# Layer 1 in pairs of tiles with seven block products each, layer 2's weights in layer 1's places, and a cosine without the absolute value

## What is computed

```python
X = rfft(x, axis=1)                  # x: 2 x 3008 x 256, an FFT layer with a complex 256x256 mix
Yr, Yi = Xr @ w_r - Xi @ w_i + b_r, Xr @ w_i + Xi @ w_r + b_i
Y = soft_threshold(Yr, 0.01) + 1j * soft_threshold(Yi, 0.01)
x = irfft(Y).reshape(6016, 256)
h = x @ w_in;  x = (h * cos(h)) @ w_out                        # layer 1: 256 -> 2048 -> 256
h = x @ w_in2; y = (h * clip(h + 3, 0, 6) / 6) @ w_out2        # layer 2: 256 -> 2048 -> 256
```

## Time and profile before

| | us |
|---|---|
| median of 3 runs (1182.27 to 1183.05) | 1182.86 |
| the profiled execution | 1183.26 |
| its span from first to last instruction | 1181.2 |
| PE busy | 1166.5 |
| ACT, DVE, POOL busy | 773.1, 760.9, 748.8 |
| mean granted TensorE clock | 0.998 of full speed |

### The profile page before, as it was taken

How to read it: one execution, slowest core, us unless ns; L and a number is a source line. 1 busy time by engine, 2 the same in 40 slices (tenths; PEclk the granted TensorE clock), 3 DMA queues, 4 the chain that set the end, 5 groups by cost and what they waited for, 6 DMA issues and landing times.

```text
span 1181.2 us, 15354 instructions
## 1 busy us (share of the span) xinstructions
PE 1166.5 (99%) x5432; PEld 985.4 (83%) x5432; DVE 760.9 (64%) x827; ACT 773.1 (65%) x1100; POOL 748.8 (63%) x505
## 2 busy tenths in 40 slices
PE   8999979999999999999999999999999999999998
PEld 8888869888888888888888888888888888888898
DVE  2777826677777777777777766565465465555544
ACT  2677656656666666666666667767667676676665
POOL 2577656556767777565677559957657557557544
PEclk9999999999999999999999999999999999999999
DMA  9375537100100100101010021020010100100000
GB/s 251 124 199 156 139 90 277 32 19 18 36 19 19 36 18 19 36 32 54 23 36 1 18 67 41 1 73 1 12 61 1 37 36 1 67 1 1 37 1 32
DMA packets 32793, 62.58 MB, mean 53 GB/s; under 512 B 3585, under 2 KB 11393, under 8 KB 32568
## 3 DMA queue, kind: packets, MB, share of 16 engines
q1 hardware_dynamic: 32718, 61.61, 16.9%
HBM read 37.22 MB, written 24.48 MB: 52 GB/s over the span
## 4 chain that ended last, share of the span: by engine, by line
PE 97%; DMA 1%; DVE 0%; ACT 0%; POOL 0%; issue 0%; SPq 0%
PE banks L627 22%; PE banks L685 22%; PE banks L644 21%; PE banks L666 19%; PE banks L519 2%; PE banks L539 2%; PE banks L535 2%; PE banks L534 2%; PE banks L592 2%; PE banks L555 1%; PE banks L554 1%; DMA v<-y_spill 1%; PE banks L504 1%; PE banks L570 0%; PE banks L567 0%; PE banks L568 0%
## 5 line engine op out<-in xcount | busy, mean ns | idle before, releaser
L1339 POOL TENSOR_TENSOR gal<-ga,gah 128x1024 fp32r<-128x1024 f32 (+1 forms) x95 | 250.0, 2632 | 174.8 <-ACT gah L897 173.3
L1420 POOL TENSOR_TENSOR gbl<-gb,gbh 128x512 fp32r<-128x512 f32 (+1 forms) x192 | 249.9, 1313 | 168.8 <-ACT gbh L1028 168.4
L889 ACT ACTIVATE cosine<-phase,half_pi 128x1024 f32<-128x1024 f32 (+1 forms) x96 | 108.8, 1133 | 132.8 <-DVE phase L1152 132.7
L1197 DVE SCALAR_TENSOR_TENSOR gb<-ramp,banks 128x512 f32<-128x512 f32 (+1 forms) x144 | 97.0, 674 | 143.1 <-ACT ramp L1021 143.1
L1170 DVE TENSOR_TENSOR ga<-banks,cosine 128x1024 f32<-128x1024 f32 (+1 forms) x96 | 115.4, 1202 | 113.4 <-ACT cosine L889 113.4
L1028 ACT ACTIVATE gbh<-gb 128x512 fp32r<-128x512 f32 (+1 forms) x192 | 118.5, 618 | 58.5 <-DVE gb L1197 57.9
L1152 DVE TENSOR_SCALAR phase<-phase 128x1024 int32<-128x1024 int32 (+1 forms) x96 | 152.7, 1590 | 3.3
L685 PE MATMUL banks<-gbh,w_lo 128*128 128x512 f32 (+1 forms) x384 | 147.9, 385 | 0.0
L685 PE MATMUL banks<-gbl,w2h 128*128 128x512 f32 (+1 forms) x384 | 147.9, 385 | 0.0
L685 PE MATMUL banks<-gbh,w2h 128*128 128x512 f32 (+1 forms) x384 | 147.9, 385 | 0.0
L666 PE MATMUL banks<-th,w2h 128*128 128x512 f32 (+1 forms) x336 | 129.4, 385 | 0.0
(11 more groups left out here) (104 smaller groups left out, 2189.6 us busy)
## 6 DMA issues: line engine op xcount, KB each, us to landing
w<-in_w_ff SPq DMA_DIRECT2D x32, 256.0 KB, 4.9
xb<-in_x SPq DMA_DIRECT2D x32, 192.0 KB, 5.7
y_spill<-y SPq DMA_DIRECT2D x24, 256.0 KB, 2.0
x<-x_spill SPq DMA_DIRECT2D x11, 512.0 KB, 4.0
x_spill<-x SPq DMA_DIRECT2D x11, 512.0 KB, 3.0
x_spill<-xs SPq DMA_DIRECT2D x11, 470.0 KB, 3.6
t<-x_spill SPq DMA_DIRECT2D x10, 512.0 KB, 4.6
out_y<-yt SPq DMA_DIRECT2D x10, 512.0 KB, 3.1
```

Of the source, the lines that this page charges most:

```text
L889: act.activation(cosine[:, :, 0:w], phase[G % 2][:, :, 0:w], ACT.Sin, bias=half_pi[:, :], scale=-1.0).then_inc(a_cos, 1)
L1339: pool.tensor_tensor(gal[G % 2][:, :, 0:w], ga[G % 2][:, :, 0:w], gah[G % 2][:, :, 0:w].bitcast(fp32), ALU.subtract).then_inc(a_gl, 1)
L1420: pool.tensor_tensor(gbl[n % RING][:, 0:w], gb[n % G_BUFS][:, 0:w], gbh[n % RING][:, 0:w].bitcast(fp32), ALU.subtract).then_inc(b_gl, 1)
```

## The change

- Layer 1 keeps the old form for its first two tiles (16 steps). The other ten are taken as five duos, 40 steps of the layer-2 kind, ahead of layer 2's six duos. In these 40 steps a block goes through `take_turns2` (ACT), `take_angle2` (DVE), `take_cos2` (ACT), `take_g2` (DVE), `round_gb` and `gb_low`, each 512 wide, in place. `copy_u2` is on DVE. The last two tiles' results of each duo go through `copy_y` (ACT) and `take_y` (DVE).
- The sums of layer 1's weight blocks are made in the 16 old steps: raw blocks loaded, `sum_s` on POOL, `round_s` on ACT, `s_low` on DVE, one pair a step. The first duo's data are prepared there too.
- Layer 2's eight weight pairs are loaded into layer 1's places as each comes free, in the last duo of layer 1 and the first of layer 2 (`load_w2`, `sum_w2`, `round_w2`, `w2_low`).
- The turns are made with a bias of -0.25, and the absolute value (L1152) goes, in all steps of layer 1.
- `sum_t` moves from two in step p = 1 and one each in p = 2, 3 to one each in p = 1 to 4, on DVE ahead of the last `take_angle2`. PSUM banks and the rings of buffers change (g: 8 and 6).

```diff
-STEPS1 = TILES * PAIRS
-DUOS = -(-TOKENS // (2 * TOK))
+CLASSIC = 2
+STEPS1 = CLASSIC * PAIRS
+DUOS1 = (TILES - CLASSIC) // 2
+DUOS2 = -(-TOKENS // (2 * TOK))
+DUOS = DUOS1 + DUOS2
+CHANGE, STEPS2 = DUOS1 * PAIRS, DUOS * PAIRS
...
             def load_w2(p):
-                sp.dma_start(w2f[p][:, A11:A11 + 4 * P], w_ff[NWCH + 2 * p, :, :]).then_inc(w2_in[p], 16)
-                sp.dma_start(w2f[p][:, UP2:W2COLS], w_ff[NWCH + 2 * p + 1, :, :]).then_inc(w2_in[p], 16)
+                freed(sp, 4 * (CHANGE - PAIRS + p) + 3)
+                for part in range(2):
+                    at = p * PCOLS + part * WCH
+                    sp.dma_start(w1f[:, at:at + WCH], w_ff[NWCH + 2 * p + part, :, :]).then_inc(w2_in[p], 16)
...
-                act.activation(phase[G % 2][:, :, 0:w].bitcast(i32), bank[:, at:at + 2, 0:w], ACT.Copy,
-                               scale=1.0 / (2.0 * math.pi)).then_inc(a_turns, 1)
+                act.activation(phase[G % 2][:, :, 0:w].bitcast(i32), bank[:, at:at + 2, 0:w], ACT.Identity,
+                               bias=quarter[:, :], scale=1.0 / (2.0 * math.pi)).then_inc(a_turns, 1)
...
+            for s in range(CHANGE):                      # ACT
+                q, p = divmod(s, PAIRS)
+                keep_u1(s)
...
+                    take_cos2(s - 1, 3)
+                keep_u5(s)
+                take_turns2(s, 0)
...
+                    round_gb(s - 1, 3)
+                if s == 1:
+                    copy_x2(1)
+                prepare2(s)
+                take_cos2(s, 0)
+                take_turns2(s, 1)
+                round_gb(s, 0)
+                take_turns2(s, 2)
+                take_cos2(s, 1)
+                take_cos2(s, 2)
+                round_gb(s, 1)
+                take_turns2(s, 3)
+                if p == 0 and q >= 1:
+                    copy_y(q - 1, 0)
+                    copy_y(q - 1, 1)
+                round_gb(s, 2)
...
-                dve.wait_ge(a_angle, G + 1)
-                bits = angle[:, :, 0:w].bitcast(i32)
-                dve.tensor_scalar(bits, bits, 0x7FFFFFFF, None, ALU.bitwise_and).then_inc(a_abs, 1)
...
+            def take_angle2(s, i):
+                n = 4 * s + i
+                dve.wait_ge(b_turns, n + 1)
+                g = gb[n % RING_G]
+                dve.scalar_tensor_tensor(out=g[:, :], in0=g[:, :].bitcast(i32), scalar=-2.0 * math.pi,
+                                         in1=h_block(s, i), op0=ALU.mult, op1=ALU.add).then_inc(b_angle, 1)
+
+            def take_g2(s, i):
+                n = 4 * s + i
+                dve.wait_ge(b_cos, n + 1)
+                g = gb[n % RING_G]
+                dve.tensor_tensor(g[:, :], h_block(s, i), g[:, :], ALU.mult).then_inc(b_g, 1)
...
+            for s in range(CHANGE):                      # DVE
+                q, p = divmod(s, PAIRS)
+                take_c11(s)
...
+                    take_g2(s - 1, 3)
+                copy_u2(s)
+                take_angle2(s, 0)
+                take_c12(s)
+                take_g2(s, 0)
+                take_c22(s)
+                take_angle2(s, 1)
+                take_angle2(s, 2)
+                take_g2(s, 1)
+                take_g2(s, 2)
+                prepare2(s)
+                take_angle2(s, 3)
+                if p == 0 and q >= 1:
+                    take_y(q - 1, 2)
+                    take_y(q - 1, 3)
```

More of the change, by code:

```diff
@@ L127, in mixer_program @@
         three = small.place("three", [P, 1], fp32)
+        quarter = small.place("quarter", [P, 1], fp32)
         sine_table = small.place("sine_table", [P, 1], fp32)
@@ L173, in mixer_program @@
         assert r.at <= nc.sbuf_usable_end
-        w2h, w2f, w2l = [None] * PAIRS, [None] * PAIRS, [None] * PAIRS
+        r = Region(v_at)
+        sh, sf, sl = [None] * PAIRS, [None] * PAIRS, [None] * PAIRS
+        for p in range(PAIRS):
+            sh[p] = r.place(f"sh{p}", [P, 4 * P], f32r)
+        for p in range(PAIRS):
+            sf[p], sl[p] = twice(r, f"s{p}", [P, 4 * P])
+        x2 = r.place("x2", PAIR, fp32)
+        ga1_at = r.at
+        ga.append(r.place("ga1", PAIR, fp32))
+        gbh_at = r.at
@@ L176, in mixer_program @@
+        xs.append(Region(gbh_at).place(f"xs{SBUF_X}", [P, DC, SPILL], fp32))
+        raw = [r.place(f"raw{i}", [P, 4 * P], fp32) for i in range(RAWS)]
+        assert r.at <= w1_at
+        r = Region(gbh_at)
+        gbh = [r.place(f"gbh{i}", ONE, f32r) for i in range(RING_H)]
+        assert r.at <= w1_at
         th, tf, tl = [None] * 2, [None] * 2, [None] * 2
[L177 to L180, removed]
+        r = Region(work_at)
@@ L192, in mixer_program @@
[L192 to L213, removed]
+        tf[0], tl[0] = twice(r, "t0", [P, 7, TOK])
@@ L214, in mixer_program @@
+        u1, u2, u5 = r.place("u1", ONE, fp32), r.place("u2", ONE, fp32), r.place("u5", ONE, fp32)
+        c22 = r.place("c22", ONE, fp32)
+        gb, gbl = [None] * RING_G, [None] * RING_G
+        gb[0], gbl[0] = twice(r, "gb0", ONE)
+        assert r.at <= nc.sbuf_usable_end
+        r = Region(u_at)
+        for i in range(1, 5):
+            gb[i], gbl[i] = twice(r, f"gb{i}", ONE)
+        yt = r.place("yt", [P, 2, DC, TOK], fp32)
+        assert r.at == phase_at
         th[1] = r.place("th1", [P, 7, TOK], f32r)
@@ L215, in mixer_program @@
         tf[1], tl[1] = twice(r, "t1", [P, 7, TOK])
+        gb[7], gbl[7] = twice(r, "gb7", ONE)
         assert r.at <= v_at
+        r = Region(ga1_at)
+        for i in range(5, 7):
+            gb[i], gbl[i] = twice(r, f"gb{i}", ONE)
         bank = ctx.enter_context(nc.psum_tensor("banks", [P, 8, 512], fp32))
@@ L1258, in _ @@
                 take_angle(G + 1)
-            for s in range(STEPS2):
+                prepare1(G)
+            for s in range(CHANGE):
                 q, p = divmod(s, PAIRS)
@@ L1268, in _ @@
                 take_gb(s, 2)
-                if p == 0 and q >= 1:
+                if p == 0:
                     take_y(q - 1, 0)
```

550 lines of the change are left out of this document (307 added, 243 removed).

## The result

The kernel after takes 1185.02 us (median of 14 runs, 1182.44 to 1185.69), the kernel before, beside it, 1182.49 (14 runs, 1181.64 to 1183.44). The ratio is 1.0019, 95% interval 1.0011 to 1.0027: the change costs about 0.2%, where 1176 was forecast, 0.6% less. The profiled execution took 1185.33 us with a span of 1183.5, against 1183.26 and 1181.2 of before: +2.3 us in the span.

A forecast was written before the change was run, and what follows sets the result against it. PE, busy in 99% of the span, was taken to bound the kernel. Sum: 1183.26 - 27.2 (matmuls) + 18.1 (duo stalls) + 0.5 (old steps) + 1.6 (layer change) = 1176.3, less 0.4 for the median: 1176 us; range 1160 to 1191.

The forecast's parts named there:

- the 120 matmuls and their pace: Layer 1's ten tiles on PE: 1800 matmuls instead of 1920, at 0.2267 us each, 27.2 us less.
- the stalls of the duos: Layer 1's five duos: loops above PE's 10.2 us make PE stall, 3.3 us a usual duo, 18.1 in all.
- The 1.3 extra of the last duo: Last layer-1 duo, steps 5 to 7: five `round_w2` and a `w2_low` add 1.3 us to its 3.3.
- the sums slip in ahead of POOL: Rival: in p = 1 to 3 DVE's `sum_t` goes before POOL's remainder; 1164 us; chance 0.28, shared with stalls smaller still.
- every loop is longer: Rival: hand-overs and POOL's lock cost 0.5 us more in each of forty steps; 1190 us, slower; chance 0.16.
- The duo's preparation lies in steps of 5.4 us with room.: First duo's data prepared in the old steps ahead of step 0: room enough, no cost put in the sum.
- the change of layers: Step 40: four `round_w2` and a cosine ahead of `keep_u2` make it late for p7, 1.6 us.
- Steps 43 to 46 ... nothing, at most 0.2 each.: Steps 43 to 46: four extra roundings where before had three with 0.7 us to spare; at most 0.2 each.
- The clock: Rival: granted clock falls after PE stalls; called small, stalls being at most 1.7 us in a 10.2 step; no chance given.
- Old steps: The 16 old steps: `sum_s` puts four instructions, 2.1 us, on POOL; stall 0 to 1.4 us, 0.5 taken.
- The cosine: Layer 1's turns: dropping DVE's absolute value is worth nothing by itself; the bias's 83 ns are hidden in old steps.
- something at the seams is late: Rival: weights or first duo's data late by one or two steps, 1186 us at most; chance 0.12 with the space between.

The follow-up runs named there:

- Experiment 5: Kernel after with `sum_t` of duos 1 to 5 replaced by writes of zeros that read nothing: 1172.02 us, ratio to before 0.9911.
- 6: Kernel after with `sum_t` moved behind `take_angle2` of block 3, all work kept: 1172.60 us, ratio to before 0.9914.
- experiment 1: Kernel after with T4's remainder made on DVE after step 13 instead of on POOL: 1179.63 us, ratio to before 0.998.
- experiment 2: Kernel after with `w2_low` of the second weight pair ahead of step 40's own ramps on DVE: 1180.05 us, ratio to before 0.9981.
- Experiment 4: Kernel after with 13 useless matmuls filling PE's wait ahead of step 0: 1183.01 us, ratio to before 1.0008.
- experiment 7: Kernel before with only the turns' bias of -0.25 and no absolute value: 1182.41 us, ratio to before 0.9999.
- experiment 8: Kernel after with T4's remainder on DVE, the second pair's `w2_low` earlier and `sum_t` later: 1163.49 us, ratio to before 0.9837.
- experiment 9: Kernel of experiment 8 with `w2_low(0, 2)` moved between step 39's angles of blocks 1 and 2: 1162.88 us, ratio to before 0.9835.

## Why the prediction was wrong

**Right: the 120 matmuls and their pace.** 5312 are there, 12 of them in 2.72 us. 27.2 us went off PE.

**Right, a little large: the stalls of the duos.** The mechanism is as worked out: POOL goes in between the g of c22 and `sum_t`, PE waits on `keep_u5`, and p = 6 catches up (9.73). Experiment 5 shows that it is this exclusion and 6 that it is this place. Forecast were 18.1 us; the five duos have 14.7 in their loops and 2.1 at the end of the last, 16.8. The usual duo has 2.6 where 3.3 was worked out. The forecast's longest loops, 11.2 and 11.7, were 11.1 and 11.1; its loop at p = 5, 9.8, was 10.8; there the lateness of p = 4 seems still to be handed on (PE's longest wait on `keep_u5`, 1.2 us, lies in that step). The 1.3 extra of the last duo was put on ACT's roundings; it was 0.3 in the loop and 2.1 as one wait for DVE's `w2_low` at the start of step 40. The rival in which the sums slip in ahead of POOL is out, by the 1.80; so is the one in which every loop is longer, by p = 6 and 7.

**The step that failed: "The duo's preparation lies in steps of 5.4 us with room."** It was never followed instruction by instruction, as the steady loop was. PE's steps of 5.4 us had room on DVE, but not on POOL: g's remainder and two `t_low` fill 5.0 to 5.3 us of each, and POOL runs without a break from 238.68 to 257.91. T4's rounded copy was there at 249.86, but its remainder stood last in that queue, behind the remainder of g 14, and step 0 waits for all seven. 6.1 us in the profiled execution (3.1 of wait, the rest behind it), where nothing was put down; experiment 1 gives back 5.4.

**The same at the change of layers.** The forecast followed ACT through step 40 and found `keep_u2` late by 1.6; it was late by about 0.4 (done at 691.27, p7 at 691.32, 5.85 us into the step where 5.44 were due). It stopped there. DVE's order in step 40, with `w2_low` of the next pair behind the four `take_y`, was not followed. Steps 40 and 41 cost 6.0; experiment 2 gives back 5.0. That the loads themselves are hidden was right: nothing there waits for a DMA.

**"Steps 43 to 46 ... nothing, at most 0.2 each."** 2.1 us. The sentence counted ACT's four roundings. The cost is on DVE, where the two `w2_low` of a step stand beside `sum_t` or `t_low` and POOL goes in between them: 1.78 us each. No experiment changed this stretch alone; the cause is read from the timeline.

**The clock was called small.** The reasoning, that stalls of 1.7 us in 10.2 cost no clock, held for the duos (the granted clock is 1.00 in each 20 us from 440 to 500). It did not ask about a longer wait, because none was in the sum. Once there were two, of 3.1 and 3.7 us, they brought 2.8 and 1.7 us of half clock with them in the profiled execution (behind the second, eight matmuls in 3.38 us from 700.68, where 1.81 were due). In the other kernels' executions the same two gaps brought 0.1 to 1.7 and 1.7 to 2.7. Why they differ stays open. Experiment 4 shows by its medians that keeping PE at work in the first gap is worth 2.0 us.

**Old steps: 0.5 us forecast, 0 found.** There the four small sums of POOL take 1.9 us, near the 2.1 worked out, and PE is busy 4.00 of 4.00 us in each stretch from 200 to 220 us.

**The cosine: right.** Nothing, shown by experiment 7.

So the rival that came true is "something at the seams is late", with the upper end given for it, 1186. The order that made it true is in the code of two queues. Its two seams, 12.1 us with their half clock against 1.6 in the sum, and the 2.1 of steps 44 to 46 are 12.6 more than forecast; 1.3 less in the duos, 0.5 less in the old steps and 1.4 less in the FFT layer leave 9.4; between the 1176.3 of the sum and the profiled 1185.33 there are 9.0. What is left are the 8.3 us between the gain of experiment 8 and the full 27.2. Its `keep_u1` distances place nearly all of them: 1.6 in the first duo, 3.0 in the fifth and 3.4 in the sixth (83.19, 84.62 and 85.02 less 81.6). Of the fifth's and sixth's, 2.3 are the wait at step 40 that experiment 9 only moved and 1.7 the half clock behind it; some 2.1 of the sixth's are steps 45 to 47 as above. The 1.6 of the first duo lie in its first two steps (11.56 and 10.41 against 20.4 for both); they and the rest were not taken apart.

## What to carry to other kernels

A steady loop can be worked out well from rows; the seams between two loops need the same work, instruction by instruction on every engine, and above all: what stands ahead, in its engine's order, of each operand that the first matmul of the new phase waits for, and whether that engine has any idle time left before it. Where DVE and POOL both work with two inputs from SBUF, put a filler of DVE behind the instruction that others wait for, and never two such instructions in a row in front of one. A wait of PE of 2.1 to 3.8 us cost its own length here and, in eleven of sixteen cases in the profiled executions, 1.7 to 2.8 us more of half clock behind it.

## What the runs showed of the hardware

- After a gap of 3.1 us PE ran twelve matmuls at 0.43 us from start to start (258.58 to 263.70), with no idle time in between, before it was back at 0.2267 (granted clock 0.53 from 260 to 264).
- The same gap cost 2.8, 1.7, 1.7 and 0.1 us of slow matmuls in four executions, and the clock behind it read 0.53, 0.76, 0.66 and 1.00 from 260 to 264 us. Waits of 2.10, 2.23 and 2.27 us were followed by half clock (behind the last 0.58 from 668 to 672 us, 1.7 us lost), waits of 2.11 to 2.18 us at the same place in four executions were not, and neither were those of up to 1.2 us in the duos. With thirteen matmuls without use in the gap the median was 2.0 us lower.
- DVE instructions that read two SBUF tensors, and stand back to back while POOL has work, take 1.78 us each instead of 0.69, one POOL instruction going in before each. A DVE write that reads nothing (485 ns) in the same place isn't held up.
- The same four sums, 0.6 us of DVE work each, cost a duo 2.6 us of stall in one place and 0.15 one instruction later. POOL's own rows are the same in both, 3.00 us for its two remainders.
